# Moving the first expert slot's choice of tokens from behind the attention stage into its last two turns

## The reference, cut to what matters

```python
# 1. attention of 8 x 8 heads, S=512 tokens and 32 state rows each, both directions
a  = softmax(scale * x @ state.T);  xread = a @ state
a2 = softmax(scale * state @ x.T);  sread = a2 @ x
x = concat([xread, sread], axis=2)  # as 4608 rows of 512
# 2. mixture of 8 experts, one expert for a token
logits = (x / |x|) @ (emb / |emb|).T / tau
expert_idx = argmax(logits);  gate_w = softmax(logits)[expert_idx]
out[mask] = gate_w * (relu(x[mask] @ w1[e]) @ w2[e])      # for each e
# 3. a last layer pair
h = out @ w_in;  g = max(h, 0) + alpha * min(h, 0);  result = g @ w_out
```

## Time and profile before

| what | value |
|---|---|
| median of 3 runs | 1362.72 us (1361.45 to 1363.45) |
| the profiled execution's own time | 1367.19 us |
| its span, first to last instruction | 1365.4 us |
| TensorE busy | 1339.8 us, 98% of the span |
| VectorE, ScalarE, GpSimd busy | 843.3, 425.0, 166.2 us |
| mean granted TensorE clock | 0.991 of full speed |

### The profile page before, as it was taken

How to read it: one execution, slowest core, us unless ns; L and a number is a source line. 1 busy time by engine, 2 the same in 40 slices (tenths; PEclk the granted TensorE clock), 3 DMA queues, 4 the chain that set the end, 5 groups by cost and what they waited for, 6 DMA issues and landing times.

```text
span 1365.4 us, 22360 instructions
## 1 busy us (share of the span) xinstructions
PE 1339.8 (98%) x7818; PEld 1155.7 (85%) x7819; DVE 843.3 (62%) x1108; ACT 425.0 (31%) x611; POOL 166.2 (12%) x228
## 2 busy tenths in 40 slices
PE   8999899999989999998999999999999999999998
PEld 7888688888878888887999999999978888888887
DVE  6899752226474444438667777678866666666652
ACT  6887431113343232325111221013322222222211
POOL 3564112121222122221000000000000000000000
PEclk9999899999999999998999999999999999999999
DMA  8884371115465425335334333434444444444453
GB/s 272 281 289 157 118 248 42 42 39 177 142 220 207 169 69 230 100 108 185 135 133 146 123 128 125 147 131 145 143 116 116 116 115 115 115 115 116 122 117 53
DMA packets 180258, 193.41 MB, mean 142 GB/s; under 512 B 24832, under 2 KB 130304, under 8 KB 179712
## 3 DMA queue, kind: packets, MB, share of 16 engines
q1 hardware_dynamic: 172960, 172.41, 40.2%
q0 software_dynamic: 6112, 19.93, 4.2%
q10 hardware_dynamic: 1152, 0.66, 0.2%
HBM read 125.07 MB, written 67.37 MB: 141 GB/s over the span
## 4 chain that ended last, share of the span: by engine, by line
PE 90%; DVE 6%; issue 1%; DMA 1%; ACT 1%; DVEq 0%; POOL 0%; ACTq 0%; SPq 0%; POOLq 0%
PE ps_p L403 13%; PE ps_p L405 13%; PE ps_p L404 13%; PE ps_h L403 5%; PE ps_h L405 5%; PE ps_h L404 5%; PE ps_y L403 5%; PE ps_o L404 5%; PE ps_o L405 5%; PE ps_y L405 5%; PE ps_o L403 5%; PE ps_y L404 5%; PE ps_hT L1651 2%; PE ps_xT L1645 1%; DVE a L1084 1%; PE ps_sr L1535 1%
## 5 line engine op out<-in xcount | busy, mean ns | idle before, releaser
L403 PE MATMUL ps_p<-b_hi,w_hi 128*128 128x272 f32 x896 | 259.5, 290 | 3.9 <-DVE b_lo L1369 3.9
L405 PE MATMUL ps_p<-b_hi,w_lo 128*128 128x272 f32 x896 | 259.5, 290 | 0.0
L404 PE MATMUL ps_p<-b_lo,w_hi 128*128 128x272 f32 x896 | 259.5, 290 | 0.0
L403 PEld LDWEIGHTS ps_p<-b_hi,w_hi 128*128 128x128 f32 x896 | 169.5, 189 | 4.9 <-DVE b_lo L1369 4.9
L405 PEld LDWEIGHTS ps_p<-b_hi,w_lo 128*128 128x128 f32 x896 | 169.8, 190 | 0.0
L404 PEld LDWEIGHTS ps_p<-b_lo,w_hi 128*128 128x128 f32 x896 | 169.3, 189 | 0.0
L1307 DVE COPY hid<-ps_h 128x512 f32<-128x512 f32 x72 | 49.8, 692 | 168.7 <-PE ps_h L405 164.6
L403 PE MATMUL ps_h<-w_hi,xgT_hi 128*128 128x512 f32 x296 | 121.7, 411 | 2.0 <-DVE xgT_lo L1178 2.0
L403 PE MATMUL ps_y<-w_hi,hidT_hi 128*128 128x512 f32 x296 | 123.5, 417 | 0.0
L1436 DVE SCALAR_TENSOR_TENSOR neg<-gt,alpha 128x2048 f32<-128x2048 f32 x33 | 75.6, 2292 | 71.6 <-DMA gt<-acts 71.6
L1447 DVE TENSOR_TENSOR g_lo<-gt,g_hi 128x2048 fp32r<-128x2048 f32 x34 | 77.9, 2292 | 65.5 <-ACT g_hi L975 65.5
(11 more groups left out here) (259 smaller groups left out, 2349.2 us busy)
## 6 DMA issues: line engine op xcount, KB each, us to landing
acts<-gb SPq DMA_DIRECT2D x128, 272.0 KB, 2.1
stage<-in_moe_w SPq DMA_DIRECT2D x32, 1024.0 KB, 5.4
gt<-acts SPq DMA_DIRECT2D x32, 1024.0 KB, 6.1
xN_all<-in_xN SPq DMA_DIRECT2D x8, 1024.0 KB, 6.2
rows_x<-xrow SPq DMA_DIRECT2D x32, 256.0 KB, 2.6
out_rows<-orow SPq DMA_DIRECT2D x32, 256.0 KB, 2.0
yz<-rows_y SPq DMA_DIRECT2D x30, 256.0 KB
xs_all<-in_xT SPq DMA_DIRECT2D x7, 1024.0 KB, 6.7
```

The lines of the kernel that those rows point to most:

```text
L403: pe.matmul(out, s_hi, m_hi, start=start, stop=False)
L404: pe.matmul(out, s_hi, m_lo, start=False, stop=False)
L405: return pe.matmul(out, s_lo, m_hi, start=False, stop=stop)
```

## The change

Work for the first slot moves forward, and other work takes its places. On ScalarE the root of the embeddings' norms moves into turn 7, between two copies of scores and the Exp. On VectorE the norms, `emb_w`, the logits of the first 16 tiles and `first_hot` move into turn 7 in front of the sums of the state softmax; ranks and places of the first slot come right behind turn 7. On TensorE the two rank matmuls move behind the turning of the last a2, the 16 place matmuls in front of the last token reads; `transpose_x(0)` comes in front of the tail's scores, the first two of four steps of `hidden(0)` in front of the ranks of all tokens; the six unread products go. On GpSimd the gather is issued ahead of the last four additions of logits. Half-chunks of weights change places: (2, first half) leaves turn 7 for the stretch behind the choice, (2, second half) follows the last choice, (3, first half) moves to the end of the index lists.

```diff
@@ PSUM places
-        ps_first_rank, ps_first_count = [ps_turn[:, 0, i * FT:(i + 1) * FT] for i in range(2)]
-        ps_first = ps_turn[:, 0, 2 * FT:2 * FT + 2]
+        ps_first_rank, ps_first_count = [ps_x[:, 0, XE + E + i * FT:XE + E + (i + 1) * FT] for i in range(2)]
+        ps_first = ps_x[:, 0, XE + E + 2 * FT:XE + E + 2 * FT + 2]
@@ gpsimd
+            def first_gather():
+                pool.wait_ge(zero_stored, 16)
+                for i in range(SC):
+                    pool.wait_ge(x_stored[i], 16 * (FT // SC))
+                pool.wait_ge(gather_ready, 1)
+                pool.indirect_dma_start(xg[:], None, rows_x[0:FT * P + 1, :],
+                                        bass.IndirectOffsetOnAxis(gather_idx[:, 0:1], 0)).then_inc(gathered, 16)
...
                     round_half(chunk, par)
+                if ending:
+                    first_gather()
                 for c in range(SC):
...
-            turn(B, 0, split=False)
...
+            turn(B, 0, split=False, ending=True)
@@ scalar
                     copy_s2(b, 1)
+                    if ending:
+                        act.wait_ge(norm_clamped, 1)
+                        act.activation(nrm[:, XT:TE], n2c[:, XT:TE], ACT.Sqrt).then_inc(norm_root, 1)
...
             copy_tr(B - 1, (2, 3))
-            act.wait_ge(norm_clamped, 1)
-            act.activation(nrm[:, XT:TE], n2c[:, XT:TE], ACT.Sqrt).then_inc(norm_root, 1)
             for c in range(SC):
                 x_rows(B - 1, c, False)
+            x_hi(1)
             for c in range(SC):
                 x_squares(B - 1, c, False, junk_late)
...
-            round_chunk(3, 3, 1, 0)
-            x_hi(1)
             act.wait_ge(h_ready, 1)
             act.activation(hid[:, 0, :], ps_h[0][:], ACT.Copy).then_inc(h_copied, 1)
-            act.wait_ge(in_slot_ready, 1)
-            act.activation(marks[:, 1, :, :, :], in_slot[:], ...).then_inc(marks_ready, 1)
+            round_chunk(3, 3, 1, 0)
             act.wait_ge(h_ready, 2)
             act.activation(hid[:, 1, :], ps_h[1][:], ACT.Copy).then_inc(h_copied, 1)
             for c in range(2):
                 hT_hi(0, c)
+            act.wait_ge(in_slot_ready, 1)
+            act.activation(marks[:, 1, :, :, :], in_slot[:], ...).then_inc(marks_ready, 1)
@@ vector
+            def expert_weights():
+                dve.wait_ge(const_cast, 8)
+                dve.wait_ge(const_loaded, 32)
+                dve.wait_ge(norm_root, 1)
+                norms(XT, TE)
+                step(dve.reciprocal(rtau[:], tau[:]))
+                step(dve.tensor_scalar(emb_w[:], ninv[:, XT:TE], rtau[:, 0:1], None, ALU.mult))
+                logits_x(0, FT)
+                most(0, FT)
+                dve.tensor_tensor(first_hot[:], lg[:, 0:FT, 0], lmax[:, 0:FT], ALU.is_equal).then_inc(first_hot_ready, 1)
+            def first_ranks():
+                dve.wait_ge(first_ranked, 1)
+                step(dve.tensor_tensor_scan(first_incl[:], ps_first_count, zeros[:, 0:FT], 0.0, ALU.add, ALU.add))
+                step(dve.tensor_tensor(first_rank[:], ps_first_rank, first_incl[:], ALU.add))
+                step(dve.tensor_scalar(first_off[:], first_incl[:, FT - 1:FT], float(P), -1.0, ALU.min, ALU.mult))
+                step(dve.tensor_scalar(first_rank[:], first_rank[:], first_off[:, 0:1], None, ALU.add))
+                step(dve.tensor_tensor(first_pos[:], first_rank[:], first_hot[:], ALU.mult))
+                for i in range(2):
+                    k = slice(i * FT // 4, (i + 1) * FT // 4)
+                    dve.tensor_tensor(place[:, k, :, :], lanes_below.unsqueeze(1).to_broadcast(half),
+                                      pairs(first_pos[:])[:, k, :].unsqueeze(2).to_broadcast(half), ALU.is_equal)\
+                       .then_inc(first_placed, 1)
...
                                       .to_broadcast([P, SC * H, NS]), ALU.subtract).then_inc(s1_sub, 1)
+                    if ending:
+                        expert_weights()
                     dve.wait_ge(s2_exp, 2 * b + 2)
...
                     if ending:
...
-                        rest_half(2, 2, 0, 0)
+                        lane_numbers()
                         copy_srow(b)
...
             turn(7, 1, ending=True)
-            rest_half(2, 2, 0, 1).then_inc(w_lo_ready, 1)
+            first_ranks()
             for k in range(2):
                 dve.wait_ge(tr_copied, 4 * (B - 1) + k + 3)
...
-            step(dve.reciprocal(rtau[:], tau[:]))
             copy_srow(B)
...
             dve.wait_ge(first_summed, 1)
...
+            logits_x(FT, XT - SC)
+            most(FT, XT - SC)
             choice(0, XT - SC)
+            step(dve.tensor_scalar(offset[:, 0:1], first_off[:], float(P), None, ALU.add))
+            dve.wait_ge(tail_turned, 1)
+            dve.tensor_copy(tailT[:, 0, :, :], ps_tailT[:, 0, :, :]).then_inc(tail_copied, 1)
+            rest_half(2, 2, 0, 0)
+            dve.wait_ge(tail_turned, 2)
+            dve.tensor_copy(tailT[:, 1, :, :], ps_tailT[:, 1, :, :]).then_inc(tail_copied, 1)
+            x_lo(1)
             logits_x(XT - SC, XT)
...
             choice(XT - SC, NT)
-            rest_half(3, 3, 1, 0).then_inc(fourth_half_ready, 1)
+            rest_half(2, 2, 0, 1).then_inc(w_lo_ready, 1)
...
             step(dve.tensor_tensor(excl[:], ps_rank, incl, ALU.add))
-            x_lo(1)
...
             dve.tensor_tensor(scatter_idx[:], idx_f[:], empty[:], ALU.add).then_inc(index_ready, 2)
+            rest_half(3, 3, 1, 0).then_inc(fourth_half_ready, 1)
             rest_half(3, 3, 1, 1).then_inc(w_lo_ready, 1)
@@ tensor
             for k in range(2):
                 turn_probs(B - 1, 1, k, False)
+            pe.wait_ge(x_copied, SC * (B - 1))
+            first_products()
             read_state(B - 1, 1, range(H // 2), False)
             for k in range(2, 4):
                 turn_probs(B - 1, 1, k, False)
             read_state(B - 1, 1, range(H // 2, H), False)
...
             for t in range(FT):
                 k = t // 2
                 pe.wait_ge(first_placed, 4 * k // FT + 1)
                 mm = pe.matmul(ps_first, place[:, k, :, t % 2], first_marks[:, t, :], start=(t == 0), stop=(t == FT - 1))
             mm.then_inc(first_summed, 1)
             pe.wait_ge(stE_copied, B)
...
-            for _ in range(6):
-                pe.matmul(ps_h[0][:], w_hi[0][:, 0:P], w_hi[0][:, 0:DM], start=True, stop=True)
+            for c in range(SC):
+                if c == 1:
+                    pe.wait_ge(gather_ready, 1)
+                read_tokens(B - 1, 1, c, False)
+                if c == 0:
+                    turn_tail(0)
+            pe.wait_ge(x_copied, SC * (B - 1) + 3)
+            transpose_x(0)
+            tail_scores(0)
+            turn_tail(1)
+            tail_scores(1).then_inc(tail_logits, 1)
+            pe.wait_ge(w_lo_ready, 2)
+            pe.wait_ge(xT_lo_ready, 1)
+            hidden(0, range(0, 2), 0)
             pe.wait_ge(sr_copied, B)
+            pe.wait_ge(x_copied, SC * B)
             pe.wait_ge(onehot_ready, 2)
             pe.matmul(ps_rank, lower[:], onehot[:], start=True, stop=True)
             pe.matmul(ps_count, ones[:], onehot[:], start=True, stop=True).then_inc(ranks_ready, 1)
-            transpose_x(0)
-            pe.wait_ge(w_lo_ready, 2)
-            pe.wait_ge(xT_lo_ready, 1)
-            for c in range(2):
-                hidden(c, range(KD), 0).then_inc(h_ready, 1)
+            hidden(0, range(2, KD), 0).then_inc(h_ready, 1)
+            hidden(1, range(KD), 0).then_inc(h_ready, 1)
```

More of the change, by code:

```diff
@@ L1195, in _ @@
-            step(dve.tensor_tensor(first_rank[:], ps_first_rank, first_incl[:], ALU.add))
-            step(dve.tensor_scalar(first_rank[:], first_rank[:], first_off[:, 0:1], None, ALU.add))
-            step(dve.tensor_tensor(first_pos[:], first_rank[:], first_hot[:], ALU.mult))
-            pairs = lambda ap: ap.rearrange("p (k r) -> p k r", r=2)
-            half = [P, FT // 4, P, 2]
-            for i in range(2):
-                k = slice(i * FT // 4, (i + 1) * FT // 4)
-                dve.tensor_tensor(place[:, k, :, :], lanes_below.unsqueeze(1).to_broadcast(half),
-                                  pairs(first_pos[:])[:, k, :].unsqueeze(2).to_broadcast(half), ALU.is_equal)\
-                   .then_inc(first_placed, 1)
@@ L1639, in _ @@
             mm.then_inc(first_summed, 1)
[L1640 removed]
+            pe.wait_ge(stE_copied, B)
             def transpose_x(s):
```

122 lines of the change are left out of this document (48 added, 74 removed).

## The result

The changed kernel takes 1367.01 us, median of 20 runs (1362.21 to 1370.19). The kernel before takes 1364.12 us, median of 20 (1361.45 to 1367.28). The ratio is 1.002, with an interval of 1.0011 to 1.0028. I had forecast 1361.6 with a range up to 1364.4, a gain of 1.1 us taken off the median shown, 1362.72. The kernel became slower, by 2.9 us between the medians, and the time lies outside the range. The median shown came from three runs; over twenty it is 1364.12, so 1.4 us of the miss of 5.4 us come from the small sample.

The account below looks back on a forecast made before the run. TensorE is full behind the choice, so the second slot's start, reached through the first slot's short path and VectorE's queue, counts. Index sums 2.2 us earlier less a 1.2 us weight half; 1.1 us off 1362.72 gives 1361.6, range 1358.7 to 1364.4.

Parts of the forecast that it names:

- The sum's base: Whole kernel: profiled 1367.19 less 1.1 gives 1366.1; the same step from the median 1362.72 gives 1361.6.
- the third half: VectorE, second slot: a weight half of 1.2 us behind the index lists cuts the 2.2 us gain to 1.0.
- The ranks: Ranks of all tokens, behind two steps of hidden: ready at 146.2 instead of 143.9.
- From the transposes to hidden: TensorE, first slot: 4.6 us (4.0 to 5.3) instead of 2.7, with tail scores, second turning and VectorE's copy between.
- Turn 7, ScalarE: Root between two table loads, 2.8 us; ScalarE catches up by the fourth xrow copy; priced at nothing.
- Turn 7, VectorE: Norms to first_hot added, 2.3 us; a2 keeps 0.7 us of cover, a1 0.2; priced at nothing.
- The port: Rival: VectorE's a1 product collides with GpSimd's stB_lo, index 0.5 us later, gain 0.6, 1362.1 us; chance 0.08.
- First index: First slot's gather_idx on VectorE: at 133.9 instead of 139.05, 5.1 us earlier.
- Gather: First slot, index to transposes: 4.4 us (4.0 to 8.0); transposes at 138.4, 6.0 us earlier.
- The late gather: Rival: landing at 7.2 us instead of 3.6 delays all behind it; 2.5 slower, 1365.2 us; chance 0.10.
- Behind the choice: Experts and last layers: TensorE full at full clock, so they gain nothing and only start earlier or later.
- the clock: TensorE's clock at 1.2 GHz by 140, back between 146 and 149.5; rivals: stays high (1360.0, chance 0.22), late (1362.5, 0.12).

Follow-up runs that it names:

- after_again: The changed kernel timed and profiled again, nothing altered: 1367.37 us, ratio 1.0029 to the kernel before.
- before_again: The kernel before, unaltered, one more profiled execution; 6.9 us at low clock, second slot at +37.1; its total time is not given.
- after_look3: The changed kernel, unaltered, one more profiled execution to see how executions differ; its total time is not given.
- scores_first: Changed kernel with the first tail scores and the second turning of the tail in front of the first slot's transposes: 1363.09 us, ratio 1.0001.
- fill_second: Changed kernel with eight unread wide products where TensorE waits for marks, in front of the index matmuls: ratio 1.0012.
- fill_both: Changed kernel with unread wide products: eight before the transposes, three before the last scores, eight before the index matmuls: ratio 1.0003.
- order_halves_fill: Changed kernel with tail scores before transposes, two weight halves moved to VectorE's idle places, eight unread products before the index matmuls: 1361.36 us, ratio 0.9986.
- more_fill: The order_halves_fill kernel with two more unread products before the transposes and three behind the last scores: ratio 0.9988.
- vector_waits: Changed kernel with VectorE's product for a1 in turn 7 waiting for GpSimd's last low state matrix: 1369.67 us, one execution.

## Why the prediction was wrong, step by step

Times behind the start of the last turning of a2:

```
                       predicted   after   after_again   before   before_again
transposes of xg         +13.3     +13.6     +12.9       +19.3      +18.8
hidden                   +17.9     +19.6     +16.7       +22.0      +21.5
scan of the ranks        +21.1     +23.1     +20.0       +18.8      +19.1
idx_h                    +31.0     +32.9     +29.8       +33.2      +30.0
second slot              +39.1     +40.7     +37.8       +40.2      +37.1
```

The 5.4 us between forecast and result are 1.4 of base (1362.72 over three runs, 1364.12 over twenty), 1.1 of a gain that did not come, and 2.9 of a loss.

**The sum's base failed.** "The same step from 1362.72" carried a gain from an execution 4.5 us above the median over to the median. But the gain was made of that execution's excess. With 13.8 us at 1.2 GHz, `hidden` ended late, and the index matmuls behind it were what `idx_h` waited for; pulling `hidden` forward promised 2.2 us there. In before_again `hidden` is faster and `idx_h` comes at +30.0. The changed kernel at its best clock has +29.8: 0.2 us of gain are left, and the third half more than takes them. I had priced it at 1.2, rightly: two halves take 2.35 us where one took 1.22. The second slot is at +37.8 and +38.1 in the two profiles with 6.6 us low, against +37.1 with 6.9 low before; with 10.1 low it is +40.7 against +39.4. That is 0.8 to 1.3 us later at like clock. Among the timed runs 38 of 91 of before have a mean clock of 0.995 (1361.9 us on average), of the 32 of the changed kernel 2 reach it (1362.3); 10 of them are at 0.990 (1369.3 us), and one of before.

**The ranks were mis-sized.** Even against the execution that it started from, the sum missed: it had the second slot at +39.1, and it stands at +40.7. I had put the ranks 2.3 us later than before. They are 4.2 later in the first profile (+23.1 against +18.8), 0.9 between the two best ones. The term behind it is "From the transposes to hidden ... I take 4.6 us (4.0 to 5.3)": 6.05 us at the low clock, outside its range, and 3.8 at the high one. At the low level the two pairs of scores took 1.71 and 1.88 us, near the 1.65 of before; but I had put the transposes and the turning at 0.5 each. Their rows are 0.63 us long in after_again, at full clock, and 1.09 here (the transposes of before had 1.11). The second pair of scores also waited 0.78 for VectorE, where I had 0.7. From the ranks on VectorE is never free: in the changed kernel's chain of waits it stands without a break from the scan to 152.30 + 0.95, and `idx_h` follows 9.9 us behind the scan (I had 9.9). So in three of the four profiles `idx_h` depends on when the ranks come, not on when `hidden` ends, and each us there arrives in full. In the fourth, after_look3, the index matmuls ran at the low level (2.67 us instead of 1.54), and `idx_h` waited for them, 11.1 us behind the scan:

```profile
158.92 0.20 DVE L1277 TENSOR_SCALAR idx_h<-ps_x 128x44 f32<-128x44 f32 x1 [1.17 <-PE ps_x L1714]
```

scores_first fits: `hidden` and the scan (142.90, +18.7) come earlier, and the whole kernel with them.

**The second pause was missed.** I had TensorE wait for `marks` and priced only its end. Behind the pause of 2.12 us at 153.16 to 155.28, a time that before was filled by `hidden`, the clock falls a second time in three of the four profiles of the changed kernel and in none of four before. Counting all runs with the pause open (2.12 to 2.65 us), it fell in six of eight profiles: not in the first of the changed kernel, and not in scores_first. In the four whose pause is filled (fill_second, fill_both, order_halves_fill, more_fill) it fell in none. fill_second, which fills it, takes 0.0017 off the ratio of after_again; the two were timed apart, each against its own runs of before, and their intervals overlap a little. I had thought of one fall only.

**Where the 3.3 us are.** The averages of all timed runs are 1363.5 us (91 runs of before) and 1366.8 us (32 of the changed kernel). Their mean clocks differ by 0.0016, 0.0016 x 2 x 1365 = 4.4 us more at 1.2 GHz. Weighing the kernels' times at like clock (0.991: 1366.6 and 1367.2; 0.992: 1364.6 and 1366.2; 0.993: 1363.0 and 1365.8; 0.994: 1364.0 and 1364.6) leaves some 1 to 1.5 us that isn't clock, and about 2 that are. This is a weighing and no proof, and the experiments don't split the loss the same way: the products of fill_both change nothing of the order, and its average is 3.1 us below after_again's (timed apart), while at like clock its executions are 2.9 us behind before (at 0.995). A mean clock counts low time also where TensorE waits (in before it is 0.50 from 144 to 148, with TensorE busy for 2.01 of the 4 us), so it isn't a measure of time lost. How the 3.3 us divide stays open. Part of the clock's share lies further back: behind the second slot's start the four profiles of the changed kernel need 1202.9 us on average, those of before 1201.3. Near 384 us, behind a pause of 3.8 to 4.3 us that both kernels have, TensorE is low for twice as long in three of four as in all four of before. The rows of before and after_again:

```profile
360.00:400.00 40.00, 35.72 (x167) 29.10 (x166) 26.92 (x29) 19.16 (x18) 9.94 (x11) 0.96 0.57 186
360.00:400.00 40.00, 36.24 (x164) 29.52 (x163) 27.10 (x29) 18.70 (x18) 8.66 (x9) 0.91 0.66 222
```

But the first profile of the changed kernel has 0.96 there, order_halves_fill has 0.91 and more_fill 1.00. That the change causes this isn't shown, and no run here separates it from chance.

**What held.** *Turn 7, ScalarE*: no cost is seen in the timeline; table loads at 116.28 and 117.81, the root at 117.58 between them. The timeline:

```profile
116.28 1.28 ACT L813 ACT_TABLE_LOAD   x1
117.58 0.21 ACT L813 ACTIVATE nrm<-n2c 128x8 f32<-128x8 f32 x1
117.81 1.28 ACT L820 ACT_TABLE_LOAD   x1
...
124.54 0.61 ACT L775 ACTIVATE xrow<-ps_x 128x528 f32<-128x528 f32 x1 [0.26 <-PE ps_x L405]
```

The root follows its load by 0.02 us. The drain of about 1.38 us that the Trainium skill adds ("ScalarE: Activation LUTs", What ACT_TABLE_LOAD costs) shows in none of these rows, and the measurement decides. *Turn 7, VectorE*: the additions took 2.3 us as predicted, and neither turning slipped. *The port*: a tie that went to VectorE. *First index*: at +8.2, predicted +8.8. *Gather*: 5.4, 4.7, 4.9 and 5.4 us from index to transposes in the four profiles, against 4.4 taken, inside 4.0 to 8.0. The late gather did not come in these four; vector_waits, with 6.7 us, shows that it can. *Behind the choice*: little moves but by the clock. Up to the end of the pause near 384 the changed kernel needs 222.0 us from its second slot and before 221.7 (profiles with a pause of 3.76 us; the clock is 1.00 from 170 to 380), 0.3 us that I did not look for.

The rival that came nearest is none of mine by itself. Its ingredients stood in the prediction: the clock, the order of the scores, and the half in the chain. Each was priced against an execution in which the other side of the choice was at its slowest.

## What to carry to other kernels

Before taking a gain off a profile, compare the profiled execution's time and mean clock with those of the timed runs: a gain found in an execution 4.5 us above the median may be only the removal of what made it long. Where two engines race for the end of a stretch, work out both sides at either level of the clock; the first layer came nearly 5 us earlier and the lists, behind the ranks, won nothing. When work is moved into a wait, put everything that does not need the awaited data in front of it, and look at what the move leaves empty: with the new pause of 2.1 us came a second fall of the clock, and with the pause filled it was gone.

## What the runs showed of the hardware

The spread of this kernel's times is not noise around one value. 91 executions of before lie between 1361 and 1367 us, and their time goes with the mean granted clock: 1361.9 us at 0.995, 1366.6 at 0.991. In the four profiles of before that difference lies mostly in one stretch of 23 us, where TensorE had thin products and pauses under 2 us. The same program was low there for 6.9, 10.1 or 13.8 us, in its changed form for 3.2 or 10.1, and no value between was seen. A second surprise is how short a pause goes before a fall: after 2.12 to 2.18 us without work, behind `hidden` and its transposes, and the narrow index matmuls, the clock fell in three of the changed kernel's four profiles. And wide products that nobody reads, put into such pauses, made no kernel here slower: fill_both has 19 of them and runs 3.2 us faster than after_again by the medians (timed apart; the ratios are 1.0003 and 1.0029), and more_fill with 13 is level with order_halves_fill with 8.
